# Transposes two tiles at a time on even steps and value products on odd steps in an attention and gated-MLP kernel

## The reference

```python
scores = scale * np.matmul(q, k.transpose(0, 1, 3, 2))
thresh = np.max(scores, axis=-1, keepdims=True) - tau
scores = np.where(scores >= thresh, scores, -1000000000.0)
scores = scores - np.max(scores, axis=-1, keepdims=True)
attn = np.exp(scores)
attn = attn / (np.sum(attn, axis=-1, keepdims=True) + 1e-09)
x = np.matmul(attn, v)
# heads side by side: x is 2304 x 512
h = x @ w_in                      # 512 -> 2048
x = (h - np.tanh(h)) @ w_out      # 2048 -> 512
h = x @ w_in2
out = (h * (1.0 / (1.0 + np.exp(-h)))) @ w_out2
```

## Time and profile before

| | |
|---|---|
| median of 3 runs | 1009.64 us (1009.54 to 1009.85) |
| the profiled execution | 1010.04 us |
| its span in the profile | 1008.2 us |
| granted TensorE clock | 0.999 |
| busy over the span | PE 98%, DVE 82%, ACT 71%, POOL 46% |
| mean of one in the attention | exponential 0.776 us, copy to pT 0.590, reduction 0.811 |
| first product of the layers | 299.98 us; the 36 of the first unit run from 300.26 to 306.50 |
| DVE's last split of x for the first pass | ends at 302.43 us |

### The profile page before, as it was taken

The page is one execution under the profiler, slowest core; times in us unless marked ns, Lnnn a source line. Parts: engine busy times, 40 slices in busy tenths (PEclk is TensorE's granted clock), DMA queues, the critical chain, the costliest instruction groups (busy, mean ns, idle before and its releaser), DMA issues.

```text
span 1008.2 us, 18094 instructions
## 1 busy us (share of the span) xinstructions
PE 990.6 (98%) x6002; PEld 900.7 (89%) x6002; DVE 828.4 (82%) x1633; ACT 716.8 (71%) x1441; POOL 463.3 (46%) x509
## 2 busy tenths in 40 slices
PE   6999999999999999999999999999999999999998
PEld 5666667676669999999999999999999999999998
DVE  7999999999988899698996989776895559935675
ACT  6999999999977766577646767387664676457643
POOL 5999999999977420264004540074201340024000
PEclk9999999999999999999999999999999999999999
DMA  6244453625213868437782577538784257734276
GB/s 213 78 180 156 168 200 135 234 93 183 88 42 118 284 216 252 146 120 274 232 250 86 197 240 248 173 105 280 220 252 167 64 188 235 246 105 168 79 254 211
DMA packets 57867, 181.00 MB, mean 180 GB/s; under 512 B 5040, under 2 KB 6576, under 8 KB 57776
## 3 DMA queue, kind: packets, MB, share of 16 engines
q1 hardware_dynamic: 57488, 179.78, 54.2%
q10 hardware_dynamic: 288, 0.07, 0.0%
HBM read 145.75 MB, written 34.08 MB: 178 GB/s over the span
## 4 chain that ended last, share of the span: by engine, by line
PE 75%; DVE 3%; issue 2%; POOL 1%; ACT 0%; ACTq 0%; POOLq 0%; DVEq 0%
PE b L1313 33%; PE b L1395 32%; PE pv L1237 4%; PE scores L1274 4%; PE tps L1296 3%; DVE g_op L1134 1%; DVE x_sum L1068 1%; POOL probs L644 1%; DVE c L1120 1%; DVE c L1103 0%; POOL w_op L598 0%; DVE b L1088 0%; POOL q_parts L665 0%; POOL k_lo L656 0%; ACT b L840 0%
## 5 line engine op out<-in xcount | busy, mean ns | idle before, releaser
L1313 PE MATMUL b<-x_op,w_op 128*128 128x384 f32 x2016 | 354.1, 335 | 0.9 <-ACT b L840 0.8
L1395 PE MATMUL b<-g_op,w 128*128 128x384 f32 x2016 | 352.6, 334 | 0.5 <-DVE g_op L1134 0.5
L1313 PEld LDWEIGHTS b<-x_op,w_op 128*128 128x128 f32 x2016 | 349.0, 188 | 4.2 <-ACT b L840 3.0
L1395 PEld LDWEIGHTS b<-g_op,w 128*128 128x128 f32 x2016 | 349.4, 188 | 2.0 <-issue 2.0
L568 POOL TENSOR_TENSOR w_sum<-w_raw 128x256 f32<-128x256 f32 x94 | 74.7, 794 | 254.8 <-PE b L1313 254.8
L977 DVE TENSOR_SCALAR_CACHE_REDUCE probs<-scores,fine 128x576 f32<-128x576 f32 x144 | 116.8, 811 | 12.8 <-PE scores L1274 12.4
L732 ACT ACTIVATE probs<-probs,stats 128x576 f32<-128x576 f32 x144 | 111.8, 776 | 19.1 <-DVE probs L1009 18.1
L882 ACT ACTIVATE g_op<-c 128x768 fp32r<-128x768 f32 x96 | 81.2, 846 | 61.0 <-DVE c L1120 34.2
L1274 PEld LDWEIGHTS scores<-k_lo,q_parts 128*128 128x128 f32 x336 | 64.0, 193 | 64.6 <-issue 38.5
L1045 DVE TENSOR_TENSOR w_op<-w_sum,w_op 128x512 fp32r<-128x512 f32 x94 | 76.0, 808 | 54.6 <-ACT w_op L795 54.3
L644 POOL TENSOR_SCALAR probs<-probs,rinv 128x576 f32<-128x576 f32 x144 | 110.1, 765 | 18.4 <-DVE rinv L1002 9.6
(11 more groups left out here) (89 smaller groups left out, 1341.3 us busy)
## 6 DMA issues: line engine op xcount, KB each, us to landing
w<-scr SPq DMA_DIRECT2D x168, 512.0 KB, 4.4
w_raw<-w_in SPq DMA_DIRECT2D x56, 512.0 KB, 3.6
scr<-w_op SPq DMA_DIRECT2D x8, 1792.0 KB, 8.6
scr<-stage SPq DMA_DIRECT2D x8, 1792.0 KB, 8.1
k_raw<-k_in SPq DMA_DIRECT2D x15, 576.0 KB, 6.1
q_raw<-q_in SPq DMA_DIRECT2D x15, 576.0 KB, 7.1
v_all<-v_in SPq DMA_DIRECT2D x16, 320.0 KB, 3.1
stage_raw<-w_in SPq DMA_DIRECT2D x8, 512.0 KB, 4.1
```

Of the source, the lines that this page charges most:

```text
L1313: last = pe.matmul(out, a, b, start=fresh and k == 0 and i == 0, stop=k == 1 and i == 2, skip_group_check=True)
L1395: last = pe.matmul(bank[n][kind], x, y, start=fresh and q == 0 and f == 0 and i == 0, stop=q == 3 and f == 1 and i == 2, skip_group_check= ...
```

## The change

PE's order is changed in the attention. At an even step it transposes the tile of that step and that of the next one; at an odd step it transposes nothing. The value products of a pair come in four bursts of 2, 3, 2, 3 blocks in place of eight bursts, all at odd steps; the lags depend on whether the pair is even or odd. ACT's copy of a finished half comes three or four steps earlier and behind the exponential of its step in place of ahead of it. The tail is three steps shorter. In the last batch of output products PE finishes one output block (n = 0) before it starts the other, and ACT's copy of the first waits for a semaphore of its own, `third_done`.

```diff
-L_PV = {L_T + 8: (0, 0, 1), L_T + 9: (0, 1, 2), L_T + 10: (0, 2, 3), L_T + 11: (0, 3, 5),
-        L_T + 12: (1, 0, 1), L_T + 13: (1, 1, 2), L_T + 14: (1, 2, 3), L_T + 15: (1, 3, 5)}
-L_OUT = {L_T + 12: 0, L_T + 16: 1}
-TAIL = (PAIRS - 1) * TILES + max(L_OUT) + 1
+L_PV = ({L_T + 6: (0, 0, 2), L_T + 8: (0, 2, 5), L_T + 10: (1, 0, 2), L_T + 12: (1, 2, 5)},
+        {L_T + 7: (0, 0, 2), L_T + 9: (0, 2, 5), L_T + 11: (1, 0, 2), L_T + 13: (1, 2, 5)})
+L_OUT = {L_T + 8: 0, L_T + 12: 1}, {L_T + 9: 0, L_T + 13: 1}
+TAIL = (PAIRS - 1) * TILES + max(L_OUT[1]) + 1
...
-TAIL_HI = (1, 1), (5, 4), (6, 6), (2, 9), (3, 10), (7, 15), (4, 18)
+TAIL_HI = (1, 1), (5, 4), (6, 6), (2, 9), (3, 10), (7, 14), (4, 18)
...
+                for k in ks:
+
+                    exponential(k)
+                    for parity, lag, a in ((i, *item) for i in range(2) for item in L_OUT[i].items()):
+                        q = k - lag
+                        if q % TILES == 0 and q // TILES % 2 == parity and here(q):
+                            p, i = q // TILES, 2 * (PAIRS * B + q // TILES) + a
+                            act.wait_ge(pv_done, i + 1)
+                            for to, of in columns(B + p // PAIRS, a):
+                                last = act.activation(xT[:, p % PAIRS, to], pv[:, of], ACT.Copy)
+                            last.then_inc(out_taken, 1)
+
+                    take_transposes(k)
...
-                act.wait_ge(batch_done, BATCHES * (z + 1))
                 for n in range(2):
+                    if z == PASSES - 1 and n == 0:
+                        act.wait_ge(third_done, 1)
+                    else:
+                        act.wait_ge(batch_done, BATCHES * (z + 1))
                     act.activation(y_tile(z, 2 + n, 0), bank[n]["21"], ACT.Copy).then_inc(y_by_act, 1)
...
+                for k in ks:
+                    scores_of(k)
+                    if k % 2 == 0:
+                        transposes_of(k)
+                        transposes_of(k + 1)
                     product(k)
+
...
+                ending = gb == BATCHES * PASSES - 1
+                for f, n in ((0, 0), (1, 0), (0, 1), (1, 1)) if ending else ((0, 0), (0, 1), (1, 0), (1, 1)):
...
+                    if ending and (f, n) == (1, 0):
+                        last.then_inc(third_done, 1)
                 last.then_inc(batch_done, 1)
```

More of the change, by code:

```diff
@@ L393, in build @@
         batch_done = sem("batch_done")
+        third_done = sem("third_done")
         p_seed_done = sem("p_seed_done")
@@ L715, in here, with take_transposes @@
                     return q < STEPS and (q >= 0 or not first)
[L717 to L733 removed]
+                def take_transposes(k):
                     for kind, q, number in units_of(k - L_T, first):
@@ L751, in steps, with exponential @@
                         last.then_inc(t_taken, 1)
+                def exponential(k):
+                    q = k - L_EXP
+                    if here(q):
+                        n, c, tile = STEPS * B + q, q % RING, probs[:, slot_of(q), :]
+                        act.wait_ge(lift_done, n + 1)
+                        act.activation(tile, tile, ACT.Exp, bias=stats[:, c, 0:1], scale=-SCALE / FINE,
+                                       accum_out=rowsum[:, c:c + 1]).then_inc(exp_done, 1)
+                for k in ks:
[9 more added lines that the diff above has]
+                    take_transposes(k)
                     if k < STEPS:
@@ L1210, in product @@
                 def product(k):
-                    for lag, (a, i0, i1) in L_PV.items():
+                    for parity, lag, (a, i0, i1) in ((i, *item) for i in range(2) for item in L_PV[i].items()):
                         q = k - lag
-                        if q % TILES == 0 and here(q):
+                        if q % TILES == 0 and q // TILES % 2 == parity and here(q):
                             p = q // TILES
@@ L1240, in product, with scores_of @@
                                 last.then_inc(pv_done, 1)
-                for k in ks:
+                def scores_of(k):
                     q = k - L_S
@@ L1389, in project @@
                 fresh = product in (1, 5)
-                for f in range(2):
+                ending = gb == BATCHES * PASSES - 1
+                for f, n in ((0, 0), (1, 0), (0, 1), (1, 1)) if ending else ((0, 0), (0, 1), (1, 0), (1, 1)):
                     g_hi, g_lo = [g_op[gb % G_SLOTS][:, i, f * TW:(f + 1) * TW] for i in range(2)]
-                    for n in range(2):
-                        hi, lo = [w2[gb % W2_SLOTS][:, f, i, n * P:(n + 1) * P] for i in range(2)]
-                        for i, (x, y) in enumerate(((lo, g_hi), (hi, g_lo), (hi, g_hi))):
-                            last = pe.matmul(bank[n][kind], x, y, start=fresh and q == 0 and f == 0 and i == 0,
-                                             stop=q == 3 and f == 1 and i == 2, skip_group_check=True)
+                    hi, lo = [w2[gb % W2_SLOTS][:, f, i, n * P:(n + 1) * P] for i in range(2)]
+                    for i, (x, y) in enumerate(((lo, g_hi), (hi, g_lo), (hi, g_hi))):
+                        last = pe.matmul(bank[n][kind], x, y, start=fresh and q == 0 and f == 0 and i == 0,
+                                         stop=q == 3 and f == 1 and i == 2, skip_group_check=True)
+                    if ending and (f, n) == (1, 0):
+                        last.then_inc(third_done, 1)
                 last.then_inc(batch_done, 1)
```

16 lines of the change are left out of this document (1 added, 15 removed).

## The result

The changed kernel takes **1011.38 us** (median, 1010.99 to 1012.27) where the kernel before takes 1009.80 on the same chip: ratio 1.0015, interval 1.0009 to 1.0020. It is slower by 1.6 us, just inside what counts as no change here (0.2%), where 1.7 us of gain was forecast. Its profiled execution took 1011.40 us with a span of 1009.6 (before: 1008.2), at a granted clock of 1.000, so the two traces can be set against each other: +1.4 us (1.46 unrounded).

The account below looks back on a forecast made before the run. POOL, full at 17.71 us a pair, was taken to bound the attention; 0 (body) - 1.3 (tail) - 0.4 (end) = -1.7 us on the median's 1009.64 gave 1007.9 us, range 1005.5 to 1012.0.

Parts of the forecast that it names:

- POOL has no room at all: Attention: POOL's idle time is all its own chain's, so it needs 17.71 us a pair, against 16.56 for DVE.
- PE is no longer a bound: Attention: with paired transposes and fewer bursts PE needs about 1.8 us less a pair.
- body 0: Saturated part of the attention: PE spends its gain waiting for norms, so 0 us, with -0.6 as bound.
- The burst that waits for ACT: Even pairs' second burst, behind ACT's "whole" copy: 0.8 us of DVE in two pairs, hidden under POOL with 1.5 left.
- PE's relief is paid out: Rival, attention: POOL has 5.5% left, so DVE's waits for scores go, 12.4 us in 260; 995.5 us, chance 0.07.
- ACT's copies behind the exponential: Attention: copies of finished halves stand behind their step's exponential and hold none back; cost 0.
- POOL is starved: Rival, attention: late reciprocals make POOL stand 0.8 us in each of seven double pairs; 1013.5 us, chance 0.17.
- The last tiles: Last four attention tiles: a stall moves to tile 139; tile 143 is reduced at 287.0, against 286.94 before; gain 0.
- The tail: From tile 143's norm to the layers: 5.7 us for 7.55, less 0.5 for ACT's queue; -1.3, bounds -1.85 and 0.
- The first pass: First pass of layers: inputs at the old times, last split of x at 302.4, its product at 305.1; 0 us.
- The end: Last output batch: the first copy is made during PE's last six products; -0.4 us, bounds 0 and -0.5.
- the one for the norm of tile 134: Sign, late attention: norm at 277 within 0.6 us; the prediction is wrong if more than a microsecond off.

Follow-up runs that it names:

- f1: Kernel before with POOL's k_lo splits cut to 64 of 576 columns from the fourth pair on: 1009.49 us, ratio 0.9999.
- e1: Changed kernel with the even pairs' value bursts and output copies two steps later: 1009.27 us, ratio 0.9994.
- f3: e1 plus the edit of e7, ACT's last split of x one step earlier, ahead of the last copy: 1008.94 us, ratio 0.9994.
- e5: Kernel before with the change's paired transposes and last batch; bursts, lags, copies and tail as before: 1022.02 us, ratio 1.0119.
- g2: e5 with ACT's copies of xT behind the exponential: 1027.31 us, ratio 1.0173.
- f4: e1 with ACT's copies of xT back ahead of the exponential: 1018.49 us, ratio 1.0088.
- e7: Changed kernel with ACT's last split of x one step earlier in the tail, ahead of its last copy: 1011.05 us, ratio 1.0010.
- e8: Changed kernel with POOL's k_lo splits cut to 64 of 576 columns from the fourth pair on: 1009.24 us, ratio 0.9992.
- e6: Changed kernel with the transposes back at every step: 1012.41 us, ratio 1.0025.
- f2: Changed kernel with DVE's last split ahead of the first pass of layers replaced by a fill with zeros: 1010.34 us, ratio 1.0007.
- e2: Kernel before with only the change's last batch of output products: 1009.29 us, ratio 0.9996.
- e3: Kernel before with one k_lo split of every odd pair moved from POOL to DVE: 1013.48 us, ratio 1.0039.
- g1: Kernel before with only ACT's copies of xT moved behind the exponential: 1018.99 us, ratio 1.0090.
- e4: Changed kernel with one k_lo split of every odd pair moved from POOL to DVE: 1013.39 us, ratio 1.0036.

## Why the prediction was wrong

Point by point, by its own steps.

*"POOL has no room at all", "PE is no longer a bound", body 0.* This is the step that failed. The sum of POOL's idle time was read rightly, but that one engine is full does not make it the one that sets the pace. The 17.71 us from norm to norm were called what POOL needs; they are the pace at which the whole attention ran. Before, DVE waited only for PE, and PE for POOL only 0.4 us, which stood in the prediction: the two kept their pace by themselves. f1 shows that POOL didn't set it. The prediction took DVE's waits for scores as slack that POOL covered; they stay (2.16 for 2.25) when POOL is relieved of 20.85 us in 180. So DVE, with the stalls that PE's order gives it, takes 35.37 us for 18 tiles by itself, POOL's work is nearly as long, and anything that adds to the stalls shows at once. The change gives 35.59, and tile 143 comes 1.54 us later.

The rule that was weighed there, of the Trainium skill ("Perfetto Trace Analysis", "Identifying the Most-Contended Engine": occupancy tells how near Vector, Scalar and GpSimd are to the limit), does not settle it here. By the windows DVE, ACT and POOL stand at 171.11, 170.07 and 170.47 of 180. Taking 20.85 us from the third is worth nothing, and three shares within 0.6% don't say which engine to relieve.

*The burst that waits for ACT: 0.8 us, hidden, "1.5 left".* The size was right to 0.03 us and the mechanism too. The cover was not there. It did not become 6.4 us either, since the stalls at tiles 3 and 17 (0.35 and 0.61) went in return: 0.83 more here and 0.40 at tile 0, but 2.47 - 2.25 = 0.22 in all. e1 and f3 take this stall away and get 0.03 and 0.07 us of 18 tiles' stall back, as it comes again in pieces; at tile 143 f3 is 1.2 us earlier. What sets that sum over all patterns is not settled: with POOL's work whole every other order tried gave 2.40 us or more, none less than before's 2.25.

*PE's relief is paid out, 995.5.* It had a chance of 0.07 and fell: PE's 10.7 us less of busy time in 180 did nothing, because what DVE waits for is not PE's mean load but what stands between two tiles' scores (e5 and g2: 3.87 and 4.63 us of stall from the order alone).

*ACT's copies behind the exponential, cost 0.* Not measured alone in the changed kernel. The prediction costed the new order with the new bursts and did not ask what the old one would cost with them: 9 us, in e1's layout (f4). The part is no detail, the new bursts need it.

*POOL is starved.* It was put down to late reciprocals; those waits stayed at 0.3 us. The new waits came from ACT's splits (L773, L771), 2.3 us in 130 tiles, small and not foreseen.

*The last tiles: 287.0.* 288.48 came: the body's lateness, and the stall of 0.83 at tile 140, where the prediction had put a harmless one at tile 139.

*The tail: -1.3 (6.2 us).* Measured -1.23 (6.32), and the closeness is partly luck. The two waits for ACT's queue were 0.61 and 0.50 us, ahead of the norm's end; they held up a burst of two blocks, so that the last transposes started 0.81 us behind that end (294.99), where 0.5 was put. PE's idle time ahead of the last burst was 0.56 in place of 0.88. The two errors cancel.

*The first pass: 0, the inputs are ahead of need.* Failed, +1.44. The prediction compared the last split (302.4) with the product that reads it, but not what DVE does next. DVE's first b comes 13.80 us behind the end of POOL's last norm before, and 13.16 in e7 and e8, where PE starts 1.2 us sooner behind that norm: DVE follows PE's start only by half, so PE finds the seed late. That takes back 0.2 us at the seed and 0.4 over the layers (e6, e7, e8), and f2, which shortens DVE's work there and loses 0.1, shows that DVE is in the path. The other microsecond stands in the changed kernel's trace alone. There the first of the pair of splits at 304.72 took 1.23 us, in every other trace 0.68 or 0.69, and 0.8 us of it is lost at the two seeds after the first. Why, and how often, stays open.

*The end: -0.4.* Measured -0.50, its bound, and -0.53 alone (e2).

So the sum was 0 - 1.3 + 0 - 0.4; measured it is 1.75 - 1.23 + 1.44 - 0.50 = 1.46 us. Of the prediction's own signs, the one for the norm of tile 134 (more than a microsecond off) came true by 0.04 us, and the transposes' waits for norms stayed under the 5 us that it named (3.4 in 180).

## What to carry to other kernels

Split every engine's idle time in waits for itself and waits for others, not only that of the engine suspected, and follow the others. Busy time plus all waits is the whole stretch for any engine and says nothing. Here POOL waited for hardly anybody, and DVE and PE only for each other; a period measured on one of them is not its need, and only a run that relieves one tells which sets the pace. A part of a change that looks like an ordering detail has to be costed with the bursts and lags it comes with, since the same order was worth -9 us in one layout and +9 in the other. One execution's trace can hold a microsecond that is not the code's; compare it at a place where both programs are still the same. And when a tail gets shorter, follow every other chain that starts at the same event up to the point where both meet again.

## What the runs showed of the hardware

DVE's subtraction of two SBUF inputs, 128x512, takes 0.68 us where POOL is idle (302.35 in the kernel before) and took 1.23 us while POOL added two SBUF inputs (304.40 and 305.47 in the changed kernel); POOL's additions took 0.99 and 1.07 us there, where 0.73 to 0.74 is their shortest in the same stretch. POOL's norm of tile 143 takes 2.07 us before and after, in place of 0.75, beside DVE's splits of x:

```profile
292.11 2.07 POOL L645 TENSOR_SCALAR probs<-probs,rinv 128x576 f32<-128x576 f32 x1 [0.49 <-DVE rinv L1011]
```

The Trainium skill, "GPSIMD Engine Reference", section "1. Specifications", says that GpSimd's way to SBUF is shared with VectorE and names VectorE's instructions with two SBUF inputs as a case of contention; these rows agree with it, in both directions.

The same k_lo split takes 1.43 us on POOL and 0.86 us on DVE (e3, median of eight). A fill of 128x768 with zeros on DVE takes 0.70 us, where the split of that size ahead of it takes 1.49 (f2).

At the start of every execution PE's 128x288 score matmuls (k_hi) took 0.44 us each, where later they took 0.29, although the profile gives a granted clock of 1.00 throughout. The moment differs from execution to execution, also with the same code: 15.7 us in e8 and f2, 16.9 in the changed kernel, 21 to 22 in e1, e7 and f3. Where the transposes come in pairs, a late moment costs time: e1, e5, e7 and f3, all at 21 us or later, reduce tile 8 at 22.65 to 23.38 us, and the changed kernel, e8, f2, f4 and g2, all by 17 us, at 22.02 to 22.16. Where they come at every step it costs nothing: before, e2, e6, f1 and g1, at 19 to 21 us, have the tile at 22.13 to 22.34. (e3 and e4 are left out, since DVE has one more split there.) This is a comparison of traces; no run was made for it.
